# Two routed expert layers after chunked attention: where GpSimd copies the gather and scatter indices within a tile's step

## Chip, core and metric

The kernel runs on one NeuronCore of one Trainium2 chip. The metric is the device time of one execution in microseconds (us). Engines are named as in the profile: PE (TensorE), DVE (VectorE), ACT (ScalarE), POOL (GpSimd) and SP (SyncE). "POOLq" is POOL's sequencer, which reads POOL's instructions in order and hands the engine its work.

## What is computed

```python
x   = chunked_attention(q, k, v)                    # 4 x 8 x 576 x 64, chunks of 64 -> x is 2304 x 512
# first mixture (m = 0), 8 experts, one expert per token
e1  = argmax(x @ w_gate)
x   = softmax(..)[e1] * sigmoid(x @ w_output_gate)[e1] * (relu(x @ w1[e1]) @ w2[e1])
# second mixture (m = 1), a router of its own, at most `capacity` tokens per expert
e2  = argmax(x @ w_gate2)
out = softmax(..)[e2] * (relu(x @ w1b[e2]) @ w2b[e2])   # 0 for a token over capacity
```

Each expert has w1 of 512 x 1024 and w2 of 1024 x 512, all float32.

## The kernel before, in words

Three stages follow each other. Attention runs over 18 blocks of 128 tokens and writes its rows to DRAM (x1). Then each mixture m is routed (tables on DVE) and run as 20 tiles of 128 rows, sorted by expert. A tile's rows are gathered from DRAM into the single tile `xg`, and its result leaves the single tile `y` by a scatter to DRAM (x2 for m = 0, out for m = 1). Gather and scatter are indirect DMAs that POOL issues; each reads its 128 row numbers from an index tile, `gidx` or `sidx`, one column of a table.

Matrix products are done on rounded parts: a weight piece (128 x 1024) comes from DRAM by an SP DMA into one of the four slots of `ring`, ACT casts it into `wh` (L600), POOL subtracts to get the rest `wl` (L427, in the function `low_parts`), and this subtraction frees the slot of `ring`. `wh` and `wl` hold two experts. An expert has 8 pieces, four for w1 and four for w2.

PE's step g is written out in this order: transposes of tile g's hidden rows (L1010), the first half of tile g+1's first product (L988 to L990), for m = 0 the transposes of result g-1 (L1029), the rest of the first product with the logits of result g-1 (L1035) between, the transposes of the gathered rows of tile g+2 (L983), and tile g's second product. The first product waits for the w1 pieces of its expert (`wl_here`), L983 for the gather of its tile (`g_in`), and L1029 for `y`.

DVE writes `y` of tile g (L830) when the second product is done and when the scatter of tile g-1 has landed (`y_out`), since there is one `y`. For m = 0 it also copies eight logits of the result into `y` (L834).

POOL's step g, the part that is changed, goes so: load three numbers from tables (L438 to L440), do the front group of weight splits (`split(lo, middle)`), scatter tile g-1, gather tile g+3, do the back group (`split(middle, hi)`). A group is empty or has four pieces here. Before each of the two DMAs stands the copy of its index column (L526 for `sidx`, L515 for `gidx`), with the waits for the transfer that used the index tile last, and the DMA waits for the copy. The waits of a DMA are carried by an instruction of their own (L264, `stand_alone`). Steps 1 to 17 are one hardware loop; steps 0, 18 and 19 are written out.

Of the kernel before, what the change touches and what calls it, by code (L numbers as in the profile page):

```python
# [23 lines left out]
def build(nc, q, k, v, wg1, wog1, w1a, w2a, wg2, w1b, w2b, cap, out):  # L24
# [29 lines left out]
    with ctx:  # L54
        def sb(name, shape, dt=F32):
            return ctx.enter_context(nc.sbuf_tensor(name, shape, dt))
# [4 lines left out]
        def sem(name):  # L61
            return ctx.enter_context(nc.semaphore(name))
# [52 lines left out]
        gather_at = [sb(f"gather_at{m}", [P, NTAB], I32) for m in range(2)]  # L115
        scatter_at = [sb(f"scatter_at{m}", [P, NTAB], I32) for m in range(2)]
# [11 lines left out]
        gidx = sb("gidx", [P, 1], I32)  # L128
        sidx = sb("sidx", [P, 1], I32)
# [100 lines left out]
        gi_here = [sem(f"gi_here{m}") for m in range(2)]  # L230
        g_in = [sem(f"g_in{m}") for m in range(2)]
        xT_done = [sem(f"xT_done{m}") for m in range(2)]
# [18 lines left out]
        si_here = [sem(f"si_here{m}") for m in range(2)]  # L251
        y_out = [sem(f"y_out{m}") for m in range(2)]
# [4 lines left out]
        def at(x, g):  # L257

            return x[:, g:g + 1] if isinstance(g, int) else x[:, bass.ds(g, 1)]
# [23 lines left out]
        def reached(t, n):  # L283

            return not isinstance(t, int) or t >= n
# [113 lines left out]
        def _(pool):  # L399
# [18 lines left out]
            def low_parts(c, slot):  # L418

                pool.wait_ge(wh_here, c + 1)  # L420
                if isinstance(c, int):
                    w = c % (2 * PX)
                    src, high, low = ring[:, slot], wh[:, w], wl[:, w]
                else:
                    one = bass.ds(c % (2 * PX), 1)
                    src, high, low = ring[:, bass.ds(slot, 1), :], wh[:, one, :], wl[:, one, :]
                nc.gpsimd.tensor_tensor(low, src, high.bitcast(F32), ALU.subtract).then_inc(wl_here, 1)  # L427
# [15 lines left out]
            def split(lo, hi):  # L443
                with pool.If(lo < hi):
                    with pool.Fori(lo, hi) as c:
                        low_parts(pool.snap(c), c % RING)
# [3 lines left out]
            def hold(instruction):  # L450

                held[0] += 1
                instruction.then_inc(g_step, 1)
                pool.wait_ge(g_step, held[0])

            for m in range(2):
                src = (x1, x2)[m]
                dst = (x2, out)[m]
                width = (ROW, D)[m]

                top = lmax[:, :].unsqueeze(2).to_broadcast([P, NT, E])
                pool.wait_ge(top_ready, m + 1)
                nc.gpsimd.tensor_tensor(lshift[:, :, :], logits[:, :, 0:E], top, ALU.subtract).then_inc(shift_ready, 1)
                if m == 0:
                    pool.wait_ge(onehot_ready, 1)
                    hold(nc.gpsimd.tensor_tensor(own[:, :, :], onehot[:, :, :],
                                                 logits[:, :, E:2 * E].rearrange("p t e -> p e t"), ALU.mult))
                    hold(nc.gpsimd.tensor_tensor(own[:, 0:4, :], own[:, 0:4, :], own[:, 4:8, :], ALU.add))
                    hold(nc.gpsimd.tensor_tensor(own[:, 0:2, :], own[:, 0:2, :], own[:, 2:4, :], ALU.add))
                    nc.gpsimd.tensor_tensor(oz[:, :], own[:, 0, :], own[:, 1, :], ALU.add).then_inc(z_ready, 1)  # L470
                pool.wait_ge(r_exp, (1, 3)[m])
                hold(nc.gpsimd.tensor_tensor(lexp[:, :, 0:4], lexp[:, :, 0:4], lexp[:, :, 4:8], ALU.add))
                hold(nc.gpsimd.tensor_tensor(lexp[:, :, 0:2], lexp[:, :, 0:2], lexp[:, :, 2:4], ALU.add))
                hold(nc.gpsimd.tensor_tensor(gsum[:, :], lexp[:, :, 0], lexp[:, :, 1], ALU.add))
                hold(nc.gpsimd.tensor_scalar_add(gsum[:, :], gsum[:, :], 1e-9))
                if m == 0:
                    pool.wait_ge(r_exp, 2)
                    hold(nc.gpsimd.tensor_scalar_add(oz[:, :], oexp[:, :], 1.0))
                    hold(nc.gpsimd.tensor_tensor(gsum[:, :], gsum[:, :], oz[:, :], ALU.mult))
                pool.sem_inc(gsum_ready, 1)  # L480
                pool.wait_ge(gate_whole, m + 1)
                hold(nc.gpsimd.tensor_copy(part[:, 0, :], gate[:, :]))
                hold(nc.gpsimd.tensor_tensor(rest[:, :], gate[:, :], part[:, 0, :], ALU.subtract))
                hold(nc.gpsimd.tensor_copy(part[:, 1, :], rest[:, :]))
                nc.gpsimd.tensor_tensor(part[:, 2, :], rest[:, :], part[:, 1, :], ALU.subtract).then_inc(gate_ready, 1)

                def gather_first(g):
                    if reached(g, 1):
                        pool.wait_ge(g_in[m], g * 16)
                        pool.wait_ge(xT_done[m], g)  # L490
                    stand_alone(pool)
                    nc.gpsimd.indirect_dma_start(xg[:, 0:src.shape[1]], None, src,
                                                 bass.IndirectOffsetOnAxis(ap=gather_at[m][:, g:g + 1], axis=0),
                                                 bounds_check=N - 1, oob_is_err=False).then_inc(g_in[m], 16)

                if m == 0:
                    for u in range(XS):
                        pool.wait_ge(x_out[u], 16 * (NT // XS))
                pool.wait_ge(index_ready, m + 1)
                gather_first(0)  # L500
                if m == 1:
                    for i in range((E + 1) * PX + PW, (E + 2) * PX):
                        low_parts(i, i % RING)
                    pool.wait_ge(s_zero, 16 * NT)
                gather_first(1)
                pool.wait_ge(routed, m + 1)
                total = tiles_of(pool, m)
                gather_first(2)

                def gather(g):  # L510

                    if reached(g, 1):
                        pool.wait_ge(g_in[m], g * 16)
                        pool.wait_ge(xT_done[m], g)
                    nc.gpsimd.tensor_copy(gidx[:, :], at(gather_at[m], g)).then_inc(gi_here[m], 1)  # L515
                    pool.wait_ge(gi_here[m], g - 2)
                    stand_alone(pool)
                    nc.gpsimd.indirect_dma_start(xg[:, 0:src.shape[1]], None, src,  # L518
                                                 bass.IndirectOffsetOnAxis(ap=gidx[:, 0:1], axis=0),
                                                 bounds_check=N - 1, oob_is_err=False).then_inc(g_in[m], 16)  # L520

                def scatter(g):

                    if reached(g, 1):
                        pool.wait_ge(y_out[m], g * 16)
                    nc.gpsimd.tensor_copy(sidx[:, :], at(scatter_at[m], g)).then_inc(si_here[m], 1)  # L526
                    pool.wait_ge(si_here[m], g + 1)
                    pool.wait_ge(y_here[m], g + 1)
                    if m == 0:
                        pool.wait_ge(yl_here, g + 1)  # L530
                    stand_alone(pool)
                    nc.gpsimd.indirect_dma_start(dst, bass.IndirectOffsetOnAxis(ap=sidx[:, 0:1], axis=0),  # L532
                                                 y[:, 0:width], None,
                                                 bounds_check=N - 1, oob_is_err=False).then_inc(y_out[m], 16)

                def step(g, ahead=True):


                    lo, middle, hi = due(m, g)
                    split(lo, middle)  # L540
                    if reached(g, 1):
                        scatter(g - 1)
                    if ahead:
                        gather(g + 3)
                    split(middle, hi)

                step(0)
                with pool.Fori(1, total - 2) as g:
                    step(g)
                step(total - 2, ahead=False)  # L550
                step(total - 1, ahead=False)
                scatter(total - 1)
                if m == 0:
                    pool.wait_ge(y_out[m], total * 16)
                    stand_alone(pool)
# [536 lines left out]
```

## Time and profile before

| what | us |
|---|---|
| median of 3 runs | 767.88 |
| lowest, highest | 763.83, 769.28 |
| the profiled execution's own time | 763.25 |
| its span, from first to last instruction | 761.4 |
| PE busy | 654.5 |
| POOL busy | 420.5 |
| DVE, ACT busy | 344.6, 170.2 |

Busy times overlap between engines, and a share of the whole span is an average over stages: attention ends at about 117 us, mixture 0's tiles run from about 134 to 437 us, mixture 1's from about 469 to 752 us. What ends a wait in one of these stretches is read from the timeline and from the chain of waits there.

### The profile page before, as it was taken

The page shows a single profiled execution, that of the slowest core. Times are in us where ns is not written, and L with a number is a line of the kernel's source. Part 1 is how long each engine was busy: PE and PEld are TensorE (multiplying, and loading weights), DVE is VectorE, ACT ScalarE, POOL GpSimd, SP SyncE. Part 2 cuts the span into 40 slices and gives each one's busy share as a digit, 9 for nine tenths or more (in the row PEclk, how much of TensorE's full clock was granted, in tenths as well). Part 3 has the DMA queues.
Part 4 walks back from the last instruction along what each step waited for, and adds up shares of the span by engine and source line. Part 5 has one row for each costly group of instructions (what it writes and reads, how often), then busy time and mean ns, then how long its engine had stood idle before and what let it go on. Part 6 is the DMA issues. An engine that isn't in the chain of part 4 may idle for free.

```text
span 761.4 us, 15861 instructions
## 1 busy us (share of the span) xinstructions
PE 654.5 (86%) x4742; PEld 540.3 (71%) x4743; DVE 344.6 (45%) x634; ACT 170.2 (22%) x205; POOL 420.5 (55%) x351
## 2 busy tenths in 40 slices
PE   4799984899999999998998623999999999999553
PEld 3698973688887888887876422788888878887442
DVE  2465657345444545434433266454545354532240
ACT  1465650002230222213224200002122210233300
POOL 1355553113786638778877524116648763679760
PEclk9999996799999999999999755999999999999796
DMA  7999988011454324454455314014225533355510
GB/s 168 277 277 269 291 261 280 28 34 60 154 207 167 110 78 165 169 191 155 170 189 173 125 15 135 29 42 151 96 92 182 167 131 111 95 183 187 190 42 22
DMA packets 79694, 111.71 MB, mean 147 GB/s; under 512 B 28249, under 2 KB 46681, under 8 KB 79664
## 3 DMA queue, kind: packets, MB, share of 16 engines
q1 hardware_dynamic: 69344, 86.05, 36.7%
q0 software_dynamic: 8000, 25.17, 9.9%
q8 instruction: 21, 0.34, 0.2%
q10 hardware_dynamic: 2320, 0.07, 0.2%
q14 instruction: 9, 0.07, 0.0%
HBM read 92.48 MB, written 20.00 MB: 148 GB/s over the span
## 4 chain that ended last, share of the span: by engine, by line
PE 63%; POOL 10%; issue 9%; DVE 6%; DMA 5%; POOLq 4%; ACT 1%; SPq 0%; ACTq 0%; DVEq 0%
PE b L988 15%; PE b L989 14%; PE b L990 14%; POOL wl L427 8%; PE b L915 5%; PE b L1010 3%; PE b L937 2%; DMA qin<-in_q 2%; PE b L983 2%; PE b L1035 2%; PE b L929 2%; PE b L892 1%; PE b L884 1%; DVE owner L761 1%; POOLq L427 1%
## 5 line engine op out<-in xcount | busy, mean ns | idle before, releaser
L427 POOL TENSOR_TENSOR wl<-ring,wh (+1 forms) x128 | 302.4, 2390 | 41.1 <-ACT wh L600 21.0
L600 ACT CAST wh<-ring 128x1024 f32 (+1 forms) x112 | 112.8, 1047 | 482.4 <-PE b L990 389.8
L988 PE MATMUL b<-wh,xTh 128*128 x320 | 134.8, 421 | 5.9 <-DVE xTl L802 3.7
L988 PE MATMUL b<-wh,hTh 128*128 x320 | 132.0, 413 | 7.5 <-DVE hTl L815 7.5
L830 DVE TENSOR_SCALAR y<-b,gates 128x512 f32<-128x512 f32 x40 | 30.0, 750 | 227.1 <-PE b L990 102.5
L989 PE MATMUL b<-wh,xTl 128*128 x320 | 128.7, 402 | 0.0
L989 PE MATMUL b<-wh,hTl 128*128 x320 | 128.6, 402 | 0.0
L990 PE MATMUL b<-wl,hTh 128*128 x320 | 127.5, 398 | 0.0
L990 PE MATMUL b<-wl,xTh 128*128 x320 | 127.5, 398 | 0.0
L792 DVE TENSOR_SCALAR h<-b 128x512 f32<-128x512 f32 x80 | 54.8, 689 | 77.9 <-PE b L990 77.7
L988 PEld LDWEIGHTS b<-wh,hTh 128*128 128x128 f32 x320 | 61.5, 192 | 21.1 <-issue 7.7
L988 PEld LDWEIGHTS b<-wh,xTh 128*128 128x128 f32 x320 | 61.3, 192 | 19.2 <-issue 7.4
L990 PEld LDWEIGHTS b<-wl,hTh 128*128 128x128 f32 x320 | 61.2, 191 | 15.0
L990 PEld LDWEIGHTS b<-wl,xTh 128*128 128x128 f32 x320 | 61.2, 191 | 14.8
L989 PEld LDWEIGHTS b<-wh,hTl 128*128 128x128 f32 x320 | 61.5, 192 | 12.7
L989 PEld LDWEIGHTS b<-wh,xTl 128*128 128x128 f32 x320 | 61.5, 192 | 11.2
L518 POOL DMA_INDIRECT xg<-x,gidx x36 | 37.9, 1052 | 31.6 <-POOL gidx L515 31.6
L815 DVE TENSOR_TENSOR hTl<-b,hTh 128x512 fp32r<-128x512 f32 x80 | 52.6, 679 | 0.0
L809 DVE CAST hTh<-b 128x512 fp32r<-128x512 f32 x80 | 51.1, 680 | 0.0
L983 PE MATMUL b<-ident,xg 128*128 128x128 f32 x168 | 26.8, 284 | 25.4 <-DMA xg<-x,gidx 12.3
L532 POOL DMA_INDIRECT x<-y,sidx x20 | 20.5, 1024 | 49.8 <-DVE y L834 26.6
L431 POOL DMA_DIRECT2D x<-xrow x18 | 10.3, 570 | 64.5 <-DVE xrow L664 64.5
(142 smaller groups left out, 667.4 us busy)
## 6 DMA issues: line engine op xcount, KB each, us to landing
ring<-in_moe_w SPq DMA_DIRECT2D x128, 512.0 KB, 3.3
vin<-in_v SPq DMA_DIRECT2D x72, 64.0 KB, 4.7
x<-xrow POOLq DMA_DIRECT2D x18, 256.0 KB, 5.9
out<-zeros SPq DMA_DIRECT2D x18, 256.0 KB, 3.2
qin<-in_q SPq DMA_DIRECT2D x6, 512.0 KB, 7.3
kin<-in_k SPq DMA_DIRECT2D x6, 512.0 KB, 7.5
qin<-in_q SPq DMA_DIRECT2D x2, 384.0 KB, 8.2
kin<-in_k SPq DMA_DIRECT2D x2, 384.0 KB, 8.3
```

The costliest lines, as they stand in the source:

```text
L427: nc.gpsimd.tensor_tensor(low, src, high.bitcast(F32), ALU.subtract).then_inc(wl_here, 1)
L518: nc.gpsimd.indirect_dma_start(xg[:, 0:src.shape[1]], None, src, bass.IndirectOffsetOnAxis(ap=gidx[:, 0:1], axis=0), bounds_check=N - 1, o ...
L600: nc.scalar.copy(dst, ring[:, i % RING]).then_inc(wh_here, 1)
L792: nc.vector.tensor_scalar_max(h[:, cols], ps_h[:, cols], 0.0).then_inc((h0_here, h1_here)[half][m], 1)
L809: nc.vector.tensor_copy(hTh[:, chunks, :], ps_hT[:, half * BANK:(half + 1) * BANK].rearrange("p (c t) -> p c t", t=P)).then_inc((hTh0_here ...
L815: nc.vector.tensor_tensor(hTl[:, chunks, :], ps_hT[:, half * BANK:(half + 1) * BANK].rearrange("p (c t) -> p c t", t=P), hTh[:, chunks, :] ...
L830: nc.vector.tensor_scalar(y[:, 0:D], ps_y, at(gates[m], j), None, ALU.mult).then_inc(y_here[m], 1)
L915: last = nc.tensor.matmul(b01[e * DH:(e + 1) * DH, u * BANK + g * P:u * BANK + (g + 1) * P], src[:, n // 2 % QS, g, e, u, :], ident[:, :], ...
L983: last = nc.tensor.transpose(ps_xT[:, c * P:(c + 1) * P], xg[:, c * P:(c + 1) * P], ident[:, :])
L988: nc.tensor.matmul(dst, high, weights(wh, *wt), start=start, stop=False)
L989: nc.tensor.matmul(dst, low, weights(wh, *wt), start=False, stop=False)
L990: return nc.tensor.matmul(dst, high, weights(wl, *wt), start=False, stop=stop)
```

## The change

In every step the copy of the index column no longer stands before its DMA. `next_gather(g + 4)` and `next_scatter(g)` stand at the end of the step and fill the index tiles for the DMAs of the step after. `next_gather` waits until all gathers issued so far, the one of this step among them, have landed; `next_scatter` waits for this step's scatter. The gather keeps its wait for the transposes, the scatter its waits for `y` and the logits. Before step 0 one copy is done in advance. The number of copies is 36 + 40 before, and one more of `gidx` for each mixture after, for a tile that is never gathered.

```diff
+                def next_gather(g):
+
+                    if reached(g, 4):
+                        pool.wait_ge(g_in[m], g * 16)
+                    nc.gpsimd.tensor_copy(gidx[:, :], at(gather_at[m], g)).then_inc(gi_here[m], 1)
+
+                def next_scatter(g):
+
+                    if reached(g, 1):
+                        pool.wait_ge(y_out[m], g * 16)
+                    nc.gpsimd.tensor_copy(sidx[:, :], at(scatter_at[m], g)).then_inc(si_here[m], 1)
+
                 def gather(g):
 
-                    if reached(g, 1):
-                        pool.wait_ge(g_in[m], g * 16)
-                        pool.wait_ge(xT_done[m], g)
-                    nc.gpsimd.tensor_copy(gidx[:, :], at(gather_at[m], g)).then_inc(gi_here[m], 1)
+                    pool.wait_ge(xT_done[m], g)
                     pool.wait_ge(gi_here[m], g - 2)
...
                 def scatter(g):
 
-                    if reached(g, 1):
-                        pool.wait_ge(y_out[m], g * 16)
-                    nc.gpsimd.tensor_copy(sidx[:, :], at(scatter_at[m], g)).then_inc(si_here[m], 1)
                     pool.wait_ge(si_here[m], g + 1)
...
                     if ahead:
                         gather(g + 3)
                     split(middle, hi)
-
+                    if ahead:
+                        next_gather(g + 4)
+                    next_scatter(g)
+
+                next_gather(3)
                 step(0)
```

On POOL, in the loop of mixture 0, from the front group's last row to the back group's first, the rows stood so before (a row of L444 or L445 is the test of a group, L513 and L525 work out addresses):

```order
L525 ISA
L526 ISA [waits y_out0]
L526 COPY sidx<-scatter_at 128x1
L532 DMA x<-y,sidx 2304x520 [waits yl_here,si_here0,y_here0]
L513 ISA
L515 ISA [waits xT_done0,g_in0]
L515 COPY gidx<-gather_at 128x1
L518 DMA xg<-x,gidx 128x512 [waits gi_here0]
L444 COMPARE_AND_BRANCH
```

In the changed kernel the same place reads:

```order
L444 UNCONDITIONAL_BRANCH
L538 DMA x<-y,sidx 2304x520 [waits yl_here,si_here0,y_here0]
L524 REGISTER_ALU
L527 DMA xg<-x,gidx 128x512 [waits xT_done0,gi_here0]
L444 COMPARE_AND_BRANCH
```

The two copies are gone from between the DMAs. They stand behind the back group, at the end of the loop's body and ahead of the next step's table loads (L438, L439):

```order
L444 UNCONDITIONAL_BRANCH
L513 ISA
L514 ISA [waits g_in0]
L514 COPY gidx<-gather_at 128x1
L519 REGISTER_ALU
L520 REGISTER_ALU [waits y_out0]
L520 COPY sidx<-scatter_at 128x1
L558 ISA
L558 COMPARE_AND_BRANCH
L438 ISA
L438 TENSOR_LOAD pieces
L438 ISA x2
```

So the wait for this step's gather (on a register instruction of the sequencer, as the wait of the copy was before) comes ahead of the next step's loads and of its front group. The last place is the change from step 18 to step 19, where no gather is left; of the changed kernel:

```order
L519 REGISTER_ALU
L520 REGISTER_ALU [waits y_out0]
L520 COPY sidx<-scatter_at 128x1
L438 TENSOR_LOAD pieces
L438 ISA x2
```

There the copy with its wait for the scatter just issued moved ahead of the loads and splits of step 19; before it stood behind them.

## Rows read from the trace of the kernel before

**Rows 1.** The page: busy us of the engines, share of the span, instructions.

```profile
PE 654.5 (86%) x4742; PEld 540.3 (71%) x4743; DVE 344.6 (45%) x634; ACT 170.2 (22%) x205; POOL 420.5 (55%) x351
```

**Rows 2.** Chain of waits, 340 to 440 us: its lines, then start, us, what.

```profile
by line: POOL wl L427 28.9%; issue 25.2%; DMA x<-y,sidx 6.4%; POOL x L532 4.1%; POOLq L427 3.4%; PE b L988 3.3%; PE b L990 3.2%; PE b L989 3.1%; PE b L1035 3.0%; DMA logits<-x 3.0%; POOLq L445 2.2%; POOLq L438 2.1%; POOLq L440 2.0%; POOLq L
...
379.14 4.78 POOL wl L427 x2
387.30 0.35 POOLq L438
```

**Rows 3.** Timeline, POOL, mixture 0, steps 16 and 17: start, us, engine, line [idle before <-releaser].

```profile
374.45 9.47 POOL L427 TENSOR_TENSOR wl<-ring,wh  x4 [1.59 <-issue]
383.86 0.19 POOL L526 COPY sidx<-scatter_at 128x1 int32 x1
384.96 1.03 POOL L532 DMA_INDIRECT x<-y,sidx  x1 [0.92 <-POOL sidx L526]
385.99 0.20 POOL L515 COPY gidx<-gather_at 128x1 int32 x1
387.05 1.05 POOL L518 DMA_INDIRECT xg<-x,gidx  x1 [0.86 <-POOL gidx L515]
389.74 9.44 POOL L427 TENSOR_TENSOR wl<-ring,wh  x4 [1.65 <-issue]
```

**Rows 4.** Timeline, PE: starts of three steps, waits for y and for gathers.

```profile
371.66 1.03 PE L1010 MATMUL b<-ident,h 128*128 128x128 f32 x8
...
385.51 1.03 PE L1010 MATMUL b<-ident,h 128*128 128x128 f32 x8
...
389.36 0.65 PE L1029 MATMUL b<-ident,y 128*128 128x128 f32 x4 [1.42 <-DVE y L830]
...
401.00 1.03 PE L1010 MATMUL b<-ident,h 128*128 128x128 f32 x8
...
614.75 0.66 PE L983 MATMUL b<-ident,xg 128*128 128x128 f32 x4 [1.72 <-DMA xg<-x,gidx]
...
712.05 1.12 PE L983 MATMUL b<-ident,xg 128*128 128x128 f32 x4 [9.47 <-DMA xg<-x,gidx]
```

**Rows 5.** Waits of POOL: who waited for what, us in total, times, longest.

```profile
POOL xg L518 <- POOL gidx L515: 31.6, 36, 0.9
...
POOL out L532 <- POOL sidx L526: 14.3, 15, 1.0
...
POOL x L532 <- POOL sidx L526: 11.1, 12, 0.9
```

**Rows 6.** The gather of L518, all 36: issue to landing.

```profile
DMA to landing us min/median/max: 3.2/3.4/4.2
```

**Rows 7.** The sequencer's own instruction of L526, 736 to 741 us.

```profile
L526 POOLq ALU_OP  x1: 35/35/35, 739.8 to 739.8; - x1
```

**Rows 8.** Timeline, POOL, mixture 0: back group of step 14, last gather before step 10, end.

```profile
281.44 1.06 POOL L518 DMA_INDIRECT xg<-x,gidx  x1 [0.85 <-POOL gidx L515]
...
359.24 9.43 POOL L427 TENSOR_TENSOR wl<-ring,wh  x4
...
369.71 1.03 POOL L532 DMA_INDIRECT x<-y,sidx  x1 [0.91 <-POOL sidx L526]
...
428.56 1.02 POOL L532 DMA_INDIRECT x<-y,sidx  x1 [0.94 <-POOL sidx L526]
431.84 0.18 POOL L526 COPY sidx<-scatter_at 128x1 int32 x1 [2.25 <-DMA x<-y,sidx]
```

**Rows 9.** Timeline, POOL, mixture 1: five DMAs.

```profile
611.34 1.06 POOL L518 DMA_INDIRECT xg<-x,gidx  x1 [0.89 <-POOL gidx L515]
...
654.29 1.05 POOL L518 DMA_INDIRECT xg<-x,gidx  x1 [0.91 <-POOL gidx L515]
...
708.57 1.05 POOL L518 DMA_INDIRECT xg<-x,gidx  x1 [0.91 <-POOL gidx L515]
...
736.98 1.03 POOL L532 DMA_INDIRECT out<-y,sidx  x1 [0.94 <-POOL sidx L526]
```

## The prediction

> **What bounds the kernel now.** Read the page's busy times first. PE is busy 86% of the span, POOL 55% [rows 1]. Seen as an average, POOL has room and small delays on it should cost nothing. The chain of waits says otherwise for one stretch: between 340 and 440 us its largest part is POOL's split, 28.9%, with "issue" and POOL's sequencer beside it and each PE line near 3% [rows 2]. So there the kernel waits for POOL's own row of work, not for its busy time.
>
> The timeline shows what that row is [rows 3]. Step 16's four splits start at 374.45 and end at 383.9. The copy of `sidx` follows, then 0.92 us in which POOL does nothing, the scatter at 384.96, the copy of `gidx`, 0.86 us idle, the gather at 387.05, and the next splits at 389.74. The step takes 15.3 us, 5.8 of them between splits: 3.2 up to the gather and 2.7 behind it. PE's own step takes 13.85 us where it waits for nothing (371.66 to 385.51) and 15.5 in the next one, with a wait of 1.42 us for `y` [rows 4]; `y` waits for the landing of the scatter of 384.96. From this pair, PE loses time as soon as a scatter starts later than about 2.0 us before PE's next step. In mixture 1 nothing on PE waits for `y` so early; there PE waits for gathers, 1.72 us at 614.75 and 9.47 at 712.05 [rows 4].
>
> **What is removed.** The idle times between a copy and its DMA sum to 31.6 us for the gather, 14.3 and 11.1 for the scatter [rows 5]. Few of them are on the path, but in a step like the one above all of it is: two copies of 0.2 and waits of 0.92 and 0.86, 2.1 us in all. With the index ready, I let the scatter start 0.05 us after the last split and the gather 1.03 later, at the scatter's end. The trace has no indirect DMA that starts behind a running split, so this is bounded: at best nothing lies between, at worst each DMA still starts 0.9 us late [rows 3]. I take the value near nothing, because the sequencer can hand both over while the splits run.
>
> **What is added.** Of the 27 groups of splits that the walk below goes through, 24 stand in front of the DMAs, so the end of the step comes right behind the gather, and the new wait there is for that same gather. It lands 3.2 to 4.2 us after its start, median 3.4 [rows 6]; the DMA instruction itself covers only 1.05 of that. Two copies of 0.2 go by the side. Behind the wait stand the table loads of the next step. They begin at 387.30 in the step above [rows 2], so 2.44 us before the first split [rows 3]. Add 0.1 for the wake-up and 0.65 for the sequencer's small instructions (addresses, two copies, the loop's end), an estimate from the pieces of 0.03 to 0.12 us of which that chain is made. From gather to next split it is then 3.4 + 0.75 + 2.44 = 6.6 us where it was 2.7. The scatter, a microsecond ahead, has landed by then and adds nothing.
>
> Does such a wait really hold up the loads behind it? The copy of L526 late in mixture 1 waits for the scatter of 736.98 [rows 9]; its sequencer instruction stands at 739.8 [rows 7], when the transfer is down. In mixture 0 the like copy starts 3.3 us after its scatter of 428.56, 2.25 of them idle [rows 8]. The sequencer stands still, and nothing behind it moves.
> The Trainium skill, Perfetto Trace Analysis, section on the SWDGE DMA instruction, draws it otherwise: an instruction is pushed into a wait queue and the sequencer goes on. The time of 739.8 speaks against it for a copy whose wait is on a register instruction; it is the first rival below.
> On the landing the skill's page DMA: Bandwidth & Descriptors, section on the anatomy of a GpSimd DMA, has 2.0 us plus bytes over 436 GB/s, which makes an estimate of 2.6 for 266 KB. By that the loss below would be about 20 us instead of 33. The row with 3.4 decides.
>
> **The sum, mixture 0.** A step with a front group now takes 9.45 (splits) + 0.05 + 1.03 + 6.6 = 17.1 us instead of 15.3; PE needs 13.85. The splits of steps 3, 4, 6 and 8 come 3 to 7 us later. PE's waits for `y` in two of these steps grow, 0.4 to 2.9 and 1.2 to 2.3, so PE is 3.5 us late at step 9. There POOL has no splits and falls back on PE: the gather of 281.44 [rows 8] goes at 284.5. Then five steps with front groups follow, 5 times 17.1, and the gather of step 14 goes at 370.2. Its back group [rows 8] hides the wait, but the two copies then stand right ahead of the next scatter, which keeps its 0.9: 382.0 against 369.71. Steps 16 and 17 add two periods, the gather of step 17 goes at 417.4, and step 18's scatter at 433.5. There `next_scatter` waits for this scatter, 3.2 us, ahead of the splits of step 19 that before began 2.7 after it. The last splits end at 449.3, and the scatter behind them goes then, against 428.56 [rows 8]. The last `y` needs its landing. Mixture 0 ends 20.5 us later.
>
> **The sum, mixture 1.** Several steps here have no splits at all. The wait lies beside PE's work up to step 7. Steps 8 and 9 both have front groups: their splits end at 597.5 and 614.6, the first products wait 2.2 and 4.6 us for `wl`, the gather of 611.34 [rows 9] goes at 615.7, and PE is 6.5 late afterwards. Steps 12 and 13 have no splits, so POOL is on PE's time again: the gather of 654.29 [rows 9] goes at 660.1. Steps 14 and 15 make it 694.4. The back group of 15 and the front group of 16 run on without a gap, and the gather of 708.57, on which PE sat 9.47 us [rows 4], goes at 715.9. One more period, one more group, and the scatter of 736.98 [rows 9], on whose landing the last two results depend, goes at 749.1: 12 us later.
>
> Together 20.5 + 12 = 32.5, with nothing gained in the attention stage. Against the profiled execution's 763.25 that is 795.8. This execution lies 4.6 below the median of the runs, 767.88, so on the median's scale I predict 800. The same bookkeeping with the old constants puts the scatters of before within 0.7 us of their rows.
>
> **Bounds.** The sum reacts by about 2 us for every 0.1 between gather and split, since some 20 steps carry it. With 0.2 less in the landing, its shortest, and half the 0.65 it is +25. If besides 0.6 of the work behind the landing were hidden, 5.5 in all, it is +14, so 782. If each DMA starts 0.4 after the split instead of at once it is about +50, 818.
>
> **Rivals.** First, faster: the sequencer does go ahead of the wait, or the loads are otherwise hidden by the landing. Then the split starts 3.9 after the gather, 1.2 later than now, and 2.1 sooner for the lost idle times, 0.9 less per step; PE's losses in both mixtures shrink and the sum is about -13, 755. It decides from 4.7 us between gather and split downward. For it: 36 idle times of 0.86 that surely go [rows 5]. Against it: the sequencer's time in rows 7. Chance 0.05.
> Second, no change: the wait costs about what the index copies gave, 4.7 us from gather to split. This needs two of the 3.9 added microseconds to vanish in work that POOL had to wait for anyway, such as ACT's casts. In the stretch of rows 3 the idle time ahead of splits is put to "issue", not to ACT. 768, chance 0.07.
> Third, much slower: a DMA's hand-over by the sequencer begins only when the engine is through with its splits, so the 0.9 stays for both DMAs in spite of the copies being gone. Only additions remain, the period is 18.8, and the sum runs to some +70, 838. The trace shows no case for or against. Chance 0.12.
> My forecast has the rest, 0.76.
>
> **Range and chances.** 782 to 822 leaves out most of the first and third rivals and the outer part of the second. A measurement of this kernel tells about 1% from no change. Faster by over 1% has 0.05, within 1% 0.07, slower by over 1% 0.88.
>
> **What would show it.** Right: in steps with a front group the gather starts 1.0 to 1.1 us after the scatter, the scatter within 0.1 of the last split, the idle time ahead of L514 is about 2.4 us and released by the gather's DMA in some 30 steps, and splits start 6.6 after the gather. Steps 16 to 17 of mixture 0 take 17.1. PE's waits for `y` are near 3 us in mixture 0's second half, and mixture 1 shows waits for `wl`. Wrong: table loads that begin before the gather has landed, a step of 15.3 or less, or idle times of 0.9 ahead of the scatter in such steps.

## The result and the profile after

| | median us | runs | ratio to the kernel before |
|---|---|---|---|
| before | 765.86 | 762.29 to 769.28 | |
| changed | 818.7 | 815.9 to 823.0 | 1.0695 (1.0622 to 1.0769) |

The changed kernel is 7% slower, 52.8 us by the two medians and also by the two spans (814.2 and 761.4). The sign, the mechanism and the range of the prediction held. The size did not: 32.5 us were forecast, and the time lies near the upper end of the range.

The page of the changed kernel:

```profile
PE 675.0 (83%) x4742; PEld 554.0 (68%) x4743; DVE 343.8 (42%) x634; ACT 171.7 (21%) x205; POOL 420.6 (52%) x353
```

PE's share fell from 86% to 83%, and POOL's busy time is the same 420 us as in [rows 1]. No engine has more to do, apart from POOL's two extra copies. PE's own 20 us more are not more matmuls: the same ones ran at a lower granted clock (0.911 over the span, 0.934 before; a mean over its two levels, 2.4 GHz as 1 and 1.2 GHz as 0.5).

The chain of waits between 400 and 480 us shows what replaced the row of POOL's instructions in [rows 2]. Columns are start, us, what:

```profile
by line: POOL wl L427 20.0%; DMA x<-y,sidx 19.2%; issue 17.8%; DMA xg<-x,gidx 6.9%; DMA logits<-x 3.7%; PE b L1045 3.3%; PE b L1000 2.5%; PE b L998 2.4%; PE b L999 2.4%; PE b L1039 2.2%; DVE y L840 1.9%; POOLq L427 1.9%; POOLq L439 1.3%; PO
...
422.87 5.54 DMA xg<-x,gidx
...
428.57 0.08 POOL gidx L514
428.94 0.29 POOLq L438
...
431.32 0.08 POOL wl L427
```

Gathers are now in the chain itself. The gather of 422.87, the slowest of all, takes 5.54 us of it, then comes the copy of `gidx` (L514), and only then the table loads of the next step (L438) and its splits. In [rows 2] the loads follow the gather's issue and no landing is in the chain of the steps between 376 and 415 us.

POOL's timeline answers to [rows 3]. One step of mixture 0 with a front group:

```profile
345.42 9.45 POOL L427 TENSOR_TENSOR wl<-ring,wh  x4 [2.50 <-issue]
355.03 1.03 POOL L538 DMA_INDIRECT x<-y,sidx  x1 [0.16 <-issue]
356.36 1.04 POOL L527 DMA_INDIRECT xg<-x,gidx  x1 [0.31 <-issue]
360.43 0.18 POOL L514 COPY gidx<-gather_at 128x1 int32 x1 [3.03 <-DMA xg<-x,gidx]
...
363.30 7.07 POOL L427 TENSOR_TENSOR wl<-ring,wh  x3 [2.50 <-issue]
```

The scatter starts right behind the splits and the gather behind it, as intended. Then POOL is idle for 3.03 us, released by the gather's own transfer, and 2.50 more ahead of the splits. The step takes 17.9 us (345.42 to 363.30) instead of 15.3. The seven such steps of mixture 0 that follow directly on each other take 17.9 to 19.4, median 18.1. From the last split's end (354.87) to the next split it is 8.4 us instead of 5.8.

The sequencer's own instructions in this step, first the table load, then what carries the wait (columns: duration min/median/max in ns, then the start in us):

```profile
L438 POOLq TENSOR_LOAD <-pieces x1: 288/288/288, 360.9 to 360.9; - x1
...
L514 POOLq FUSED_REGOPS  x1: 37/37/37, 360.3 to 360.3; - x1
```

The instruction with the wait runs at 360.3 and the load behind it at 360.9, after the landing. This is [rows 7] again, now for 33 of the 36 gathers. In total:

```profile
POOL gidx L514 <- DMA xg<-x,gidx: 96.3, 33, 4.7
...
PE b L1039 <- DVE y L840: 33.6, 13, 5.0
```

33 waits of POOL for the gather it has just issued, 96.3 us together, and 13 waits of PE for `y`, 33.6 us, up to 5.0 each. Before, the second kind summed to 10.2 us.

Landing times, from the DMA's start, first of the gathers (L527), then of the scatters (L538):

```profile
DMA to landing us min/median/max: 3.3/3.8/5.5
...
DMA to landing us min/median/max: 2.6/4.0/4.6
```

[rows 6] had 3.2/3.4/4.2 for the same 36 gathers. In mixture 0 of the changed kernel the eleven gathers right behind splits land in 3.9 to 5.5 us and the seven others in 3.3 to 3.5. PE's waits, which answer to [rows 4]:

```profile
360.37 0.65 PE L1039 MATMUL b<-ident,y 128*128 128x128 f32 x4 [3.43 <-DVE y L840]
...
636.15 0.66 PE L993 MATMUL b<-ident,xg 128*128 128x128 f32 x4 [3.16 <-DMA xg<-x,gidx]
...
771.76 0.79 PE L998 MATMUL b<-wh,xTh 128*128 x1 [2.51 <-POOL wl L427]
...
795.64 0.79 PE L998 MATMUL b<-wh,hTh 128*128 x1 [9.73 <-DVE hTl L825]
```

In mixture 0 PE waits 3.43 us for `y` in this step, where [rows 4] had 1.42. In mixture 1 it waits for gathers, once for `wl`, and at the end 9.73 us for `hTl`: DVE casts tile 19's hidden rows behind `y` of tile 18, and that `y` waits for the scatter of tile 17 to land.

By stages: from mixture 0's third gather to mixture 1's third, and from there to the last scatter, the changed kernel takes 32.3 and 23.1 us more (334.53 and 270.99 us before, 366.85 and 294.13 after). What lies ahead of mixture 0's third gather, attention above all, was 2.7 us shorter in this one profile, which is within what single executions differ by.

In mixture 1 this delay has two parts. From its third gather to its last scatter PE's 1166 matmul records take 248.0 us at a granted clock of 0.97 before, and 258.4 us at 0.94 after. So 10.4 of the 23.1 us are busy time at a lower clock, and 12.7 are idle time (23.0 before, 35.7 after).

### The profile page after: what moved, and what is told of

Its sections match the earlier page's. It is cut to its first block, busy times and chain, and to the rows that moved or that the text cites. A ratio compares the mean times of both kernels' runs of the same rounds, so it can differ in the third digit from the quotient of the medians.

```text
span 814.2 us, 15857 instructions
## 1 busy us (share of the span) xinstructions
PE 675.0 (83%) x4742; PEld 554.0 (68%) x4743; DVE 343.8 (42%) x634; ACT 171.7 (21%) x205; POOL 420.6 (52%) x353
## 4 chain that ended last, share of the span: by engine, by line
PE 48%; DMA 16%; POOL 11%; issue 11%; DVE 6%; POOLq 4%; SPq 2%; ACT 1%; DVEq 0%; ACTq 0%
PE b L998 11%; PE b L999 10%; PE b L1000 10%; POOL wl L427 9%; DMA x<-y,sidx 6%; DMA xg<-x,gidx 5%; PE b L925 3%; PE b L947 2%; PE b L1020 2%; PE b L993 2%; PE b L1045 2%; DMA ring<-in_moe_w 2%; DMA out<-y,sidx 1%; PE b L939 1%; PE b L1039 1%
## 5 line engine op out<-in xcount | busy, mean ns | idle before, releaser
L998 PE MATMUL b<-wh,hTh 128*128 x320 | 135.3, 423 | 16.5 <-DVE hTl L825 16.5
L998 PE MATMUL b<-wh,xTh 128*128 x320 | 138.2, 432 | 8.1 <-DVE xTl L812 3.7
L999 PE MATMUL b<-wh,xTl 128*128 x320 | 131.5, 411 | 0.0
L999 PE MATMUL b<-wh,hTl 128*128 x320 | 131.1, 410 | 0.0
L1000 PE MATMUL b<-wl,xTh 128*128 x320 | 130.4, 407 | 0.0
L1000 PE MATMUL b<-wl,hTh 128*128 x320 | 129.9, 406 | 0.0
L998 PEld LDWEIGHTS b<-wh,hTh 128*128 128x128 f32 x320 | 63.2, 198 | 32.3 <-issue 18.4
L998 PEld LDWEIGHTS b<-wh,xTh 128*128 128x128 f32 x320 | 63.5, 198 | 22.2 <-issue 9.8
L999 PEld LDWEIGHTS b<-wh,xTl 128*128 128x128 f32 x320 | 63.6, 199 | 11.8
L514 POOL COPY gidx<-gather_at 128x1 int32 (+1 forms) x38 | 6.9, 182 | 96.3 <-DMA xg<-x,gidx 96.3
L527 POOL DMA_INDIRECT xg<-x,gidx x36 | 37.3, 1036 | 35.3 <-PE b L993 24.6
L993 PE MATMUL b<-ident,xg 128*128 128x128 f32 x168 | 27.0, 286 | 27.0 <-DMA xg<-x,gidx 13.9
L993 PEld LDWEIGHTS b<-ident,xg 128*128 128x128 f32 x168 | 21.4, 147 | 34.4 <-DMA xg<-x,gidx 15.7
```

Source lines behind the costliest of these rows:

```text
L993: last = nc.tensor.transpose(ps_xT[:, c * P:(c + 1) * P], xg[:, c * P:(c + 1) * P], ident[:, :])
L998: nc.tensor.matmul(dst, high, weights(wh, *wt), start=start, stop=False)
L999: nc.tensor.matmul(dst, low, weights(wh, *wt), start=False, stop=False)
L1000: return nc.tensor.matmul(dst, high, weights(wl, *wt), start=False, stop=stop)
```

## The experiments

All ratios are to the kernel before, run on the same chip in the same session. "M0" is the time from the first to the last scatter of mixture 0 in the one profiled execution: 269.9 us before, 302.9 in the changed kernel.

| kernel | ratio, 95% interval | M0, us |
|---|---|---|
| wait only | 1.1017 (1.0976 to 1.1059) | 307.1 |
| only gidx at the end | 1.0718 (1.0669 to 1.0766) | 298.8 |
| gather ahead of scatter | 1.0714 (1.0666 to 1.0762) | 303.3 |
| only sidx at the end | 1.0333 (1.0282 to 1.0383) | 285.2 |
| copies behind the loads | 1.0132 (1.0093 to 1.0171) | 276.0 |
| both copies ahead of the scatter | 0.9893 (0.9837 to 0.9949) | 262.4 |
| copies inside the front group | 0.9798 (0.9754 to 0.9843) | 263.6 |
| small weight transfers | one run, 791.96 us | 291.0 |

### Only the wait, nothing moved

```diff
                     split(middle, hi)
+                    if ahead:
+                        pool.wait_ge(g_in[m], (g + 4) * 16)
+                        pool.sem_inc(alone, 1)
```

The second new line only gives the wait an instruction to sit on.

> The kernel before, with its copies where they were, and one wait more: at the end of every step with a gather, POOL's sequencer waits until that gather has landed. My theory (the exposed wait is the whole loss, the earlier DMAs are a gain): a step with a front group takes 19 us, so the kernel is 75 to 85 us slower than the kernel before, and slower than the changed kernel. Rival (the changed kernel is slow because its DMAs start close behind the splits and each other, and land later): little more than before, 0 to 25 us. Landing of the gather: 3.4 us median if the extra 0.4 of the changed kernel comes from its earlier start, 3.8 if it comes from the wait.

Measured: 844.33 us against 767.01, 77 more. A step of mixture 0:

```profile
396.20 1.03 POOL L532 DMA_INDIRECT x<-y,sidx  x1 [0.93 <-POOL sidx L526]
...
398.29 1.05 POOL L518 DMA_INDIRECT xg<-x,gidx  x1 [0.85 <-POOL gidx L515]
404.48 9.44 POOL L427 TENSOR_TENSOR wl<-ring,wh  x4 [5.14 <-issue]
```

From gather to next split it is 6.2 us; before it was 2.7 [rows 3]. The copies and their idle times are as before. The wait alone thus costs more than the whole change. The landing is not disturbed:

```profile
DMA to landing us min/median/max: 3.3/3.4/4.1
```

So the later landing in the changed kernel doesn't come from the wait. It has to do with when the gather starts.

### The copies behind the next step's table loads

```diff
                     lo, middle, hi = due(m, g)
+                    if ahead:
+                        next_gather(g + 3)
+                    if reached(g, 1):
+                        next_scatter(g - 1)
                     split(lo, middle)
...
-                    if ahead:
-                        next_gather(g + 4)
-                    next_scatter(g)
...
```

The copy ahead of step 0 goes too, and one of `sidx` comes ahead of the last scatter; the next two kernels do the same.

> The changed kernel, but the two copies with their waits stand behind the three table loads of the next step and ahead of its front group, so that 2 us of sequencer work lie beside the landing. Theory of the exposed wait: from gather to next split 4.3 to 4.9 us instead of 7, near the 4.7 at which gain and loss cancel, so the time is that of the kernel before, -3 to +11 us. Rival (late landings or crowded DMAs are what costs, not the sequencer's order): it stays at +30 us or more.

Measured: 777.79 against 767.01, at the upper end of what was expected. In a step with a front group:

```profile
386.42 1.04 POOL L527 DMA_INDIRECT xg<-x,gidx  x1 [0.31 <-issue]
390.68 0.18 POOL L514 COPY gidx<-gather_at 128x1 int32 x1 [3.23 <-DMA xg<-x,gidx]
...
391.43 9.46 POOL L427 TENSOR_TENSOR wl<-ring,wh  x4 [0.37 <-issue]
```

The wait is there (3.23 us) and the DMAs start as early as in the changed kernel. But the loads are done by the time the gather has landed, and the splits start 0.4 us behind the copies. From gather to split it is 5.0 us in this step instead of 7. Two microseconds of the sequencer's work, put on the other side of one wait, are worth 42 us of the change's 53.

### The copies inside the front group

```diff
-                    split(lo, middle)
+                    split(lo, middle - 1)
+                    if ahead:
+                        next_gather(g + 3)
+                    if reached(g, 1):
+                        next_scatter(g - 1)
+                    with pool.If(lo < middle):
+                        last = pool.snap(middle - 1)
+                        low_parts(last, last % RING)
```

with nothing at the end of the step.

> The changed kernel, but the copies with their waits stand ahead of the last split of the front group (the group is cut in two for that), some 8 us behind the gather. The DMAs start as early as in the changed kernel and nothing waits for a landing. Theory of the exposed wait: no idle time ahead of the gidx copy in steps with a front group, a step of 13.9 to 14.4 us where POOL is the bound, and 14 to 18 us faster than the kernel before. Rival (crowding of the early DMAs): not faster than the kernel before.

Measured: 752.41 against 767.01, 14.6 us faster. The timeline shows the copies between the third and fourth split, with no idle time of their own:

```profile
372.50 7.08 POOL L427 TENSOR_TENSOR wl<-ring,wh  x3 [1.17 <-ACT wh L614]
...
382.35 1.03 POOL L538 DMA_INDIRECT x<-y,sidx  x1 [0.17 <-issue]
383.68 1.04 POOL L527 DMA_INDIRECT xg<-x,gidx  x1 [0.30 <-issue]
384.75 7.11 POOL L427 TENSOR_TENSOR wl<-ring,wh  x3
391.81 0.18 POOL L514 COPY gidx<-gather_at 128x1 int32 x1
...
392.07 2.37 POOL L427 TENSOR_TENSOR wl<-ring,wh  x1
394.61 1.03 POOL L538 DMA_INDIRECT x<-y,sidx  x1 [0.17 <-issue]
395.94 1.03 POOL L527 DMA_INDIRECT xg<-x,gidx  x1 [0.31 <-issue]
```

The scatter starts 0.17 us behind the last split. One gain had not been expected: the splits of 384.75 start 1.07 us behind the gather instead of 2.7. The sequencer runs the next step's table loads from 382.1 to 383.8 us here, so it has passed both DMAs before either begins. In the kernel before the loads start behind the gather, at 387.30 for the one of 387.05. The step takes 12.3 us (372.50 to 384.75), where 13.9 to 14.4 had been expected.

Most of the later splits are late for another reason now:

```profile
POOL wl L427 <- ACT wh L614: 41.3, 14, 5.1
...
POOL gidx L514 <- DMA xg<-x,gidx: 32.2, 11, 3.6
```

41.3 us of waits for ACT's casts, which wait for PE to be through with an expert: POOL has caught up with PE. The 11 waits for gathers lie ahead of steps without splits. In seven of them POOL then waits 2.6 to 8.4 us more for PE or for `y`; in the other four, all in mixture 1, the next scatter waits only for its copy. The gathers behind splits land as late as in the changed kernel (3.8 to 5.4 us in all but one in mixture 0), and the kernel is faster all the same. So DMAs that start close behind the splits do no harm where no landing is exposed; the rival of crowding falls.

### Both copies together ahead of the scatter

```diff
                     split(lo, middle)
+                    if ahead:
+                        next_gather(g + 3)
+                    if reached(g, 1):
+                        next_scatter(g - 1)
                     if reached(g, 1):
                         scatter(g - 1)
...
-                    if ahead:
-                        next_gather(g + 4)
-                    next_scatter(g)
...
```

> Both copies together ahead of the scatter, where the copy of sidx stood before, nothing at the end of the step. No wait is exposed (the gather before has landed while the splits ran), the scatter starts 0.2 us later than in the kernel before, the gather 0.6 to 0.8 us earlier. A step that POOL bounds takes 14.6 us instead of 15.3; 4 to 8 us faster than the kernel before. Rival (moving copies away from their DMA costs in itself): not faster.

Measured: 754.04 against 764.54, 10.5 us faster, somewhat more than expected.

```profile
378.37 1.03 POOL L538 DMA_INDIRECT x<-y,sidx  x1 [0.92 <-POOL sidx L520]
379.70 1.03 POOL L527 DMA_INDIRECT xg<-x,gidx  x1 [0.31 <-issue]
381.71 9.46 POOL L427 TENSOR_TENSOR wl<-ring,wh  x4 [0.98 <-ACT wh L611]
```

The scatter keeps its 0.92 us behind the copy, and the gather follows 1.33 us behind it instead of 2.09. The next loads start at 379.3, ahead of the gather, and the splits start 2.0 us behind it; ACT's casts end their last wait. The step is 14.0 us (367.74 to 381.71), below the expected 14.6.

### One copy of the two

Only `sidx` at the end of the step, the copy of `gidx` ahead of its gather with its old waits:

```diff
                     split(middle, hi)
-                    if ahead:
-                        next_gather(g + 4)
                     next_scatter(g)
```

> Only the copy of sidx at the end of the step, with its wait for this step's scatter; the copy of gidx stays ahead of its gather. Theory of the exposed wait: the scatter starts 0.9 us earlier and lands in some 3.9, which ends about 1 us after the gather's own 1.05 us; a step with a front group takes 16.3 to 16.9 us, the kernel is 15 to 30 us slower than before, about half of the changed kernel's loss. Rival (only the wait for the gather matters): no slower than the kernel before, or some us faster.

Measured: 788.51 against 764.54, 24 us more.

```profile
344.73 1.02 POOL L541 DMA_INDIRECT x<-y,sidx  x1 [0.16 <-issue]
...
346.82 1.05 POOL L530 DMA_INDIRECT xg<-x,gidx  x1 [0.87 <-POOL gidx L527]
349.11 0.18 POOL L520 COPY sidx<-scatter_at 128x1 int32 x1 [1.24 <-DMA x<-y,sidx]
351.80 9.47 POOL L427 TENSOR_TENSOR wl<-ring,wh  x4 [2.51 <-issue]
```

The scatter, early by 0.9, lands 4.3 us after its start, 1.24 us after POOL is through with the gather's issue. The step takes 16.7 us. Both lie within what was expected.

Only `gidx` at the end, the copy of `sidx` ahead of its scatter:

```diff
                     if ahead:
                         next_gather(g + 4)
-                    next_scatter(g)
```

> Only the copy of gidx at the end of the step; the copy of sidx stays ahead of its scatter, 1.1 us behind the last split. The wait for the gather is whole and only one of the two starts is gained, so a step takes 18.3 to 18.6 us and the kernel is 58 to 70 us slower than before, more than the changed kernel. Rival (the two waits add up): less than the changed kernel's 53.

Measured: 819.25 against 764.54, 55 more. That is less than the 58 to 70 expected, and the intervals of the two ratios don't tell it from the whole change.

```profile
342.81 1.03 POOL L535 DMA_INDIRECT x<-y,sidx  x1 [0.93 <-POOL sidx L529]
344.15 1.03 POOL L521 DMA_INDIRECT xg<-x,gidx  x1 [0.31 <-issue]
347.79 0.18 POOL L514 COPY gidx<-gather_at 128x1 int32 x1 [2.61 <-DMA xg<-x,gidx]
350.47 9.46 POOL L427 TENSOR_TENSOR wl<-ring,wh  x4 [2.50 <-issue]
```

The step takes 18.2 us. The gather, 2.4 us behind the last split here, has its copy 3.6 us after its start instead of 4.1. The two halves lose 24 and 55 us, 79 together, and the whole change 53. That fits two waits that end within about a microsecond of each other: the change pays only the later one, and it gains both early starts.

### Why the gather lands later

The gather's landing was sized at 3.4 us and measured 3.8. Two things are near it in the changed kernel: a scatter 1.3 us ahead, and the weight transfers of SP for the slots of `ring` that the last splits have just freed, 512 KB each and 3.3 us long. First the order of the two DMAs was turned round:

```diff
                     split(lo, middle)
+                    if ahead:
+                        gather(g + 3)
                     if reached(g, 1):
                         scatter(g - 1)
-                    if ahead:
-                        gather(g + 3)
```

> The changed kernel with the gather ahead of the scatter. It tells what made the gather's landing 3.8 us instead of 3.4. If it is the scatter 1.3 us ahead of it, the gather now lands in 3.4. If it is the weight transfers for the ring slots that the last splits have just freed, the gather, 0.2 us behind the last split, lands in 3.8 or more. The time: y waits 1.3 us longer for its scatter, so equal to the changed kernel or up to 15 us slower.

Measured: 821.46 against 767.01, 1.0714, so equal to the changed kernel. Two steps, the first with a front group, the second without one:

```profile
346.24 1.06 POOL L527 DMA_INDIRECT xg<-x,gidx  x1
347.61 1.01 POOL L538 DMA_INDIRECT x<-y,sidx  x1 [0.31 <-issue]
350.49 0.18 POOL L514 COPY gidx<-gather_at 128x1 int32 x1 [1.87 <-DMA xg<-x,gidx]
...
394.64 1.05 POOL L527 DMA_INDIRECT xg<-x,gidx  x1 [2.12 <-PE b L993]
...
398.21 0.18 POOL L514 COPY gidx<-gather_at 128x1 int32 x1 [1.19 <-DMA xg<-x,gidx]
```

With nothing of POOL's ahead of it, the gather behind the splits still takes 4.2 us to its copy (346.24 to 350.49), and the one in the step without splits 3.6, in spite of a scatter 1.4 us behind both. The scatter is not the cause. Then the weight transfers were made small, to a quarter of the columns; the other columns keep what the slot held, so the results and mixture 1's routing are other ones:

```diff
                         dst = dst.rearrange("p (b d) -> p b d", d=D)
+                        dst, w = dst[:, :, 0:D // 4], w[:, :, 0:D // 4]
+                    else:
+                        dst, w = dst[:, 0:PIECE // 4], w[:, 0:PIECE // 4]
                     sp.dma_start(dst, w).then_inc(piece_in[i % RING], 16)
```

> The changed kernel with weight transfers for experts 2 to 7 of mixture 0 and all of mixture 1 that carry a quarter of the columns; the other columns keep what the slot held, so results and the routing of mixture 1 differ and only mixture 0 is compared. If the gather lands late behind splits because the ring's transfers run beside it, the median landing in mixture 0 falls from about 4.2 us in steps with a front group to 3.4 to 3.6, and mixture 0 takes 6 to 10 us less than in the changed kernel. If it is another thing that goes with the splits, landing and time stay.

```profile
342.29 1.03 POOL L530 DMA_INDIRECT xg<-x,gidx  x1 [0.31 <-issue]
345.76 0.18 POOL L517 COPY gidx<-gather_at 128x1 int32 x1 [2.44 <-DMA xg<-x,gidx]
```

The gather's landing in mixture 0, here and in the changed kernel (min/median/max):

```profile
DMA to landing us min/median/max: 3.1/3.3/3.9
```

```profile
DMA to landing us min/median/max: 3.3/4.0/5.5
```

4.0 went to 3.3, and mixture 0, by this one profile, from 302.9 to 291.0 us, 12 less, a bit more than expected. So the weight transfers are what delays the gather behind splits. Not all of the 5.5 is theirs: the last gather of mixture 0 takes 3.9 us with the small transfers too, and 4.0 in the kernel before. The kernel with both copies together agrees: its gathers start about 2.4 us behind the last split, when most of the last weight transfer is through, and land in the old time:

```profile
DMA to landing us min/median/max: 3.2/3.4/4.0
```

## Why the prediction was right, and where it was too small

**The bound.** It was right that POOL's row of instructions sets the time from the middle of mixture 0, and that busy shares don't show it. The three kernels that only rearrange this row without an exposed wait or with less of it spread from -2% to +1.3%.

**The wait.** It was right that the wait for this step's gather holds the sequencer and all that stands behind it. The instruction at 360.3 with the load at 360.9 shows it directly, the kernel with only the wait shows that it costs 77 us by itself, and the kernel with the copies behind the loads shows that the cost lies in what stands behind the wait. The first rival (the sequencer goes on during the wait) falls with that. The section of the Trainium skill that was cited for it, Perfetto Trace Analysis on the SWDGE DMA instruction, draws the wait in a queue beside the sequencer. In this program the wait sits on a register instruction of the sequencer, and there it holds everything. Where all waits are satisfied the sequencer does go ahead, as the loads at 382.1 us in the kernel with the copies inside the front group show. The other page of the Trainium skill that was cited, DMA: Bandwidth & Descriptors, leads to an estimate of 2.6 us for the landing. The measured 3.3 to 5.5 decide.

**The break-even.** 4.7 us from gather to split was the point forecast for gain and loss to cancel. The kernel with the copies behind the loads has 4.6 to 5.4 in mixture 0 and lies at +1.3%, which fits.

**The terms that were mis-sized.** First the landing, "3.2 to 4.2 us after its start, median 3.4". It was read from gathers that started 3.2 us behind the last split. The change moves them to 1.5 us behind it, into the weight transfers, and there they take 3.9 to 5.5 in mixture 0. The scatter of step 18, sized at 3.2, lands in 4.0, and the scatters that start 0.2 us behind splits take 3.8 to 4.6 in mixture 0. PE's waits for `y` grew too. Second the starts: 0.05 us ahead of the scatter and nothing ahead of the gather were 0.17 and 0.31 each time. The third rival, 0.9 for both, was therefore wrong, but so was "at once". Third, the sequencer's part behind the landing was about 0.2 too long: from landing to split it is 3.0, and 3.2 had been allowed. From gather to split it is 6.9 to 8.5 us in mixture 0, median 7.2, instead of 6.6, and the step is 18.1 instead of 17.1. At the prediction's own 2 us for every 0.1 this one microsecond makes 20 us more, 52.5 in all. That was worked out afterwards, is no forecast, and comes out so close in part by luck, as mixture 1 shows.

**The two stages.** 20.5 and 12 us were forecast, and 32.3 and 23.1 measured. The prediction has no term for PE's clock. In mixture 1 the idle time of PE grew by 12.7 us and its busy time, at the lower clock, by 10.4. How much of the 10.4 is on the path was not separated, so this term stands beside the longer steps as a possible part of what was missing. In the second half of mixture 0 POOL's row sets the time, so PE's slower matmuls there should only shorten its waits; that was not measured.

**The range.** 818.7 lies inside mainly because the range allowed for late starts of the DMAs; what filled it were later landings as much as starts. Its lower side doesn't follow the rule of 2 us for every 0.1, by which the two favourable cases are +22 and +10 and not +25 and +14.

**The places in mixture 1.** Waits for `wl` of 2.2 and 4.6 us were forecast behind the splits of steps 8 and 9. The trace has one wait for `wl` at all, 2.51 us at 771.76. In the steps named PE waits for gathers instead (3.16 us at 636.15), and in several steps a microsecond for `hTl`. So the stage was late, as forecast, but what ends the waits on PE was not as forecast.

**What stays open.** Why 0.31 us lie between scatter and gather with both waits long satisfied was not tried. How much of the 12 us saved by small weight transfers is landing and how much is other traffic was not separated. Why the last gather of mixture 0 is slower than the others in every kernel is open as well.

## What to carry to other kernels

A wait for a DMA that is put at the end of a loop's body is a wait in front of the whole next body, address loads included; put it behind the work that doesn't need it, as far from the DMA's issue as that work allows. Moving an instruction off a critical row is only half of the edit: the other half is where its waits land, and the same index copies were worth -2% inside the splits and +7% at the end of the step. When an edit makes a transfer start earlier, look at which transfers are in flight at that new time before its old duration is used.

## What the runs showed that had not been expected

- In the changed kernel's mixture 0 an indirect gather of 128 rows lands in 3.9 to 5.5 us when it starts 1.5 us behind splits, and in 3.3 to 3.5 elsewhere. Behind splits it runs beside the 512 KB weight transfers that these let go; with transfers a quarter as large the median went from 4.0 to 3.3.
- Two indirect DMAs whose waits are long satisfied still have 0.31 us between them on POOL, and 0.17 stand between a split and a DMA. A DMA behind a copy it depends on has 0.86 to 0.96.
- With all waits satisfied POOL's sequencer had run the next step's loads before the gather ahead of them was through, and the splits followed the gather's start by 1.07 us instead of 2.7.
- Two microseconds of sequencer instructions, on one side of a wait or on the other, made 1.0695 or 1.0132 of the whole kernel's time.
